# Attention with the values as TensorE weights: the transposed output, normalised and gated behind the product

## The chip, the cores and the metric

The kernel runs on one core of a Trainium2 chip. The metric is the device time of one execution in microseconds (us), lower is better. All data are float32 in HBM at the start and at the end. TensorE multiplies (a matmul is a load of its stationary operand, the weights, and the pass of the moving one), VectorE and ScalarE work elementwise and read PSUM, GpSimd gathers and scatters, SyncE issues most DMAs. Each engine takes its instructions in program order and meets the others at semaphores.

## What is computed

Three layers one after the other: chunked attention with memory, then two mixtures of experts. The part that the change touches is the attention and the first gate:

```python
B, H, S, D = 4, 8, 768, 64          # chunk 32, 16 keys to the left, 8 to the right, 8 memory keys
for c in range(S // 32):            # per chunk: 32 queries against its 56 keys and the 8 of memory
    scores = scale * np.matmul(q_c, k_full.transpose(0, 1, 3, 2))
    a = np.exp(scores - np.max(scores, axis=-1, keepdims=True))
    a = a / (np.sum(a, axis=-1, keepdims=True) + 1e-09)
    out[:, :, c_start:c_end] = np.matmul(a, v_full)
x = out.transpose(0, 2, 1, 3).reshape(3072, 512)
logits = x @ w_gate                 # 3072 x 8; tokens are then given to experts by sorted logits
```

The first mixture gives every expert 384 of the 3072 tokens in order of the logits; the second takes the best two experts of each token.

## The kernel before, in words

Attention goes in 32 blocks of 96 queries (8 for each of the 4 batch rows) against 128 keys: 120 of the context and 8 of memory, with a mask added by a matmul. `stages` runs `step(b, i, before, after)` for each block n = 8b + i; batch rows 0 and 3 are unrolled, rows 1 and 2 are a loop of 8 unrolled steps. The work is pipelined over blocks, in each engine by an order written out by hand:

- TensorE (lines 570 to 660), in the step of block n: `turn_probs(n)` for the two head parities (r = 0, 1), `scores(n+1)` (two mask matmuls at L594, then 16 matmuls at L600, two heads in different halves of the rows), `turn_x(n-1)` (4 transposes), `turn_qk(n+2)` (4 + 4 transposes), `sums(n)` (the value product: 16 matmuls at L612, the turned probabilities are the weights, 96 columns, and the values move, 64 columns; float32 takes two matmuls each), `gate(n-1)` (8 matmuls, the gate's 8 columns as weights, 96 columns moving).
- ScalarE (L1388 to L1426): `copy_logits(n-2)`, `copy_x(n-1)` out of PSUM, the 8 exponentials of block n+1 with their row sums, `copy_q(n+2)`.
- VectorE (L905 to L953): the two copies of the turned probabilities of n, the inverse of the row sums, the two maxima of n+1, `copy_k(n+2)`, `normalise(n)` of the sums of n into x.
- SyncE (L443 to L460): the load of block n+4, five DMAs, once the value product of n is done (a ring of 4 input buffers), then the store of x of block n to `x_dram`, once it is normalised. Before the loop it loads block 0, the two gates of the second mixture, the gate `gate_w`, and blocks 1 to 3.

Before its first scores TensorE waits for the masks and for the gate weights. After block 31 it turns the logits of all tokens, kept as 8 x 3072, in 24 transposes; VectorE copies them and the routing of the first mixture begins (L1092 and on). Ahead of its last `normalise` VectorE has a chain of constants for the routing (L982 to L997). The experts' weights, the routing and everything else come behind that and are not touched.

## Time and profile before

| | us |
|---|---|
| timed runs: median of 3 (lowest, highest) | 1430.89 (1430.78, 1433.11) |
| the profiled execution | 1426.65 |
| its span, first to last instruction | 1424.9 |
| granted TensorE clock, mean over the span | 0.94 |
| busy: TensorE matmul / weight load | 1268.4 / 1125.7 |
| busy: VectorE / ScalarE / GpSimd | 952.5 / 594.2 / 294.3 |

The busy time of a TensorE row is modelled at its end, since matmuls are pipelined; the distance between the starts of two groups is the better measure of what a group takes. The span has three stages: attention to about 193 us, the first mixture with its routing to about 700, the second to the end. The profile's clock is 1.00 where the granted clock is 2.4 GHz and 0.50 where it is 1.2 GHz.

### The profile page before, as it was taken

What the parts mean: (1) busy time and instruction counts of PE and PEld (TensorE: products, weight loads), DVE (VectorE), ACT (ScalarE), POOL (GpSimd) and SP (SyncE); (2) the same over time, 40 slices, a digit from 0 to 9 for tenths busy, and PEclk for the clock granted to TensorE, in tenths of its full rate; (3) what the DMA queues carried; (4) which work ended last, traced back from release to release, by engine and by line L of the source; (5) the groups of instructions that cost most, each with busy time, mean ns of one, the idle gap of its engine ahead of it and who ended that gap; (6) DMA issues with size and microseconds to landing.
All of it is one profiled execution on the core that took longest, in us unless ns stands there. A gap on an engine that the chain in (4) does not pass through costs nothing.

```text
span 1424.9 us, 28417 instructions
## 1 busy us (share of the span) xinstructions
PE 1268.4 (89%) x9825; PEld 1125.7 (79%) x9825; DVE 952.5 (67%) x1904; ACT 594.2 (42%) x1252; POOL 294.3 (21%) x345
## 2 busy tenths in 40 slices
PE   7999962599989999889249999999999999999997
PEld 6888851478778778768149999898989999999996
DVE  4777757788888787344666666666666666666662
ACT  4666621123323323333214545444445454444541
POOL 2000000210220210220122423332323333333322
PEclk9999975599999999899659999999999999999999
DMA  8888853133333233432013425124343324252110
GB/s 144 169 161 166 169 199 120 57 123 115 102 111 113 88 123 115 144 133 72 16 46 104 133 60 177 38 82 134 94 147 117 131 81 138 72 163 87 61 32 3
DMA packets 174760, 154.62 MB, mean 109 GB/s; under 512 B 105581, under 2 KB 138349, under 8 KB 174704
## 3 DMA queue, kind: packets, MB, share of 16 engines
q1 hardware_dynamic: 151552, 102.83, 26.2%
q0 software_dynamic: 16608, 44.56, 10.1%
q10 hardware_dynamic: 6544, 6.49, 1.3%
q8 instruction: 35, 0.57, 0.2%
q14 instruction: 21, 0.17, 0.0%
HBM read 215.58 MB, written 34.28 MB: 175 GB/s over the span
## 4 chain that ended last, share of the span: by engine, by line
issue 38%; PE 31%; DVE 12%; POOL 10%; DMA 6%; ACT 2%; POOLq 1%; DVEq 0%; SPq 0%; ACTq 0%
PE bank L730 6%; PE bank L750 5%; POOL partial L400 3%; DMA out<-result,token_now 3%; PE bank L612 3%; POOL out L404 3%; DMA xg<-x_dram,token_of 3%; PE bank L621 2%; PE bank L600 2%; POOL held L382 2%; PE bank L682 2%; POOL x L386 2%; PE bank L636 2%; PE bank L696 1%; PE bank L629 1%
## 5 line engine op out<-in xcount | busy, mean ns | idle before, releaser
L536 DVE TENSOR_TENSOR w_part<-w_sb,w_part 128x1024 fp32r<-128x1024 f32 x296 | 361.1, 1223 | 113.8 <-ACT w_part L530 105.4
L530 ACT CAST w_part<-w_sb 128x1024 fp32r<-128x1024 f32 x296 | 307.0, 1046 | 215.1 <-PE bank L890 169.7
L873 PEld LDWEIGHTS bank<-x2T,w_part 128*128 128x128 f32 x2784 | 339.2, 193 | 4.0 <-DVE x2T L1332 1.8
L873 PE MATMUL bank<-x2T,w_part 128*128 128x256 f32 x2784 | 340.1, 284 | 1.4 <-DVE x2T L1332 1.4
L890 PE MATMUL bank<-w_part,h2T 128*128 128x512 f32 x1392 | 323.2, 391 | 0.0
L890 PEld LDWEIGHTS bank<-w_part,h2T 128*128 128x128 f32 x1392 | 259.2, 188 | 52.6
L750 PE MATMUL bank<-w_part,hT 128*128 128x512 f32 x576 | 155.3, 409 | 8.2 <-DVE w_part L536 8.2
L730 PE MATMUL bank<-xgT,w_part 128*128 128x384 f32 x768 | 146.4, 345 | 2.6 <-DVE hT L1040 1.8
L356 POOL DMA_INDIRECT xg<-x_dram,token_of x24 | 32.6, 1358 | 554.9 <-DVE token_of L1071 302.5
L1544 ACT ACTIVATE h2T<-bank 128x512 fp32r<-128x512 f32 x116 | 69.3, 597 | 174.8 <-PE bank L873 174.8
L730 PEld LDWEIGHTS bank<-xgT,w_part 128*128 128x128 f32 x768 | 135.8, 192 | 5.0 <-DVE hT L1040 1.6
L1338 DVE SCALAR_TENSOR_TENSOR h2T<-bank,h2T 128x512 fp32r<-128x512 f32 x116 | 80.2, 692 | 86.0 <-ACT h2T L1544 86.0
L750 PEld LDWEIGHTS bank<-w_part,hT 128*128 128x128 f32 x576 | 103.4, 190 | 28.1 <-issue 9.7
L382 POOL TENSOR_TENSOR held<-iota_p 1x1 f32<-1x1 f32 x87 | 41.3, 475 | 406.7 <-DVE result L1357 388.3
L1392 ACT ACTIVATE probs<-bank,neg_max 96x128 f32<-96x128 f32 x256 | 89.3, 368 | 7.9 <-DVE neg_max L909 7.9
L1435 ACT ACTIVATE hT<-bank 128x384 fp32r<-128x384 f32 x64 | 31.5, 492 | 126.6 <-PE bank L730 126.6
L1357 DVE SCALAR_TENSOR_TENSOR result<-bank,w_now,partial 128x512 f32<-128x512 f32 x58 | 43.4, 748 | 44.8 <-PE bank L890 44.8
L386 POOL DMA_INDIRECT x<-y_dram,slot_now x58 | 60.9, 1050 | 56.0 <-DVE slot_now L1324 38.6
L682 PEld LDWEIGHTS bank<-above,proposal 128*8 128x8 bf16 x1176 | 31.8, 83 | 51.1 <-DVE above L1115 44.1
L682 PE MATMUL bank<-above,proposal 128*8 128x32 bf16 (+1 forms) x1176 | 37.5, 177 | 38.8 <-DVE above L1115 38.8
L400 POOL DMA_INDIRECT partial<-out,token_now x58 | 62.5, 1078 | 18.6 <-issue 16.2
L404 POOL DMA_INDIRECT out<-result,token_now x58 | 59.2, 1021 | 21.6 <-POOL held L382 16.0
(256 smaller groups left out, 1341.9 us busy)
## 6 DMA issues: line engine op xcount, KB each, us to landing
w_sb<-in_moe_w SPq DMA_DIRECT2D x296, 512.0 KB
k_in<-in_k SPq DMA_DIRECT2D x32, 240.0 KB
v_in<-in_v SPq DMA_DIRECT2D x32, 240.0 KB
q_in<-in_q SPq DMA_DIRECT2D x32, 192.0 KB
x_dram<-x_sb SPq DMA_DIRECT2D x32, 192.0 KB, 3.4
out<-zeros SPq DMA_DIRECT2D x1, 6144.0 KB, 19.7
y_dram<-y_sb ACTq DMA_DIRECT2D x24, 256.0 KB, 2.0
x<-y_dram,slot_now POOLq DMA_INDIRECT x58
```

The source lines that it names most:

```text
L386: pool.indirect_dma_start(out=x2[:, par, half, :], out_offset=None, in_=y_dram[:, :], in_offset=bass.IndirectOffsetOnAxis(ap=slot_now[:, p ...
L400: pool.indirect_dma_start(out=partial[:, par, half, :], out_offset=None, in_=out[:, :], in_offset=tokens[half], bounds_check=N - 1, oob_is ...
L404: pool.indirect_dma_start(out=out[:, :], out_offset=tokens[half], in_=result[:, par, half, :], in_offset=None, bounds_check=N - 1, oob_is_ ...
L530: scalar.copy(split_part(0, c), raw_part(c)).then_inc(hi_ready[c], 1)
L536: nc.vector.tensor_tensor(split_part(1, c), raw_part(c), split_part(0, c).bitcast(F32), ALU.subtract).then_inc(lo_ready[c], 1)
L682: last = nc.tensor.matmul(counts[:, 0:bins], proposal[:, c, :], above[:, c, 0:bins], start=(c == 0), stop=(c == COLS - 1))
L730: last = nc.tensor.matmul(bank[2 + f % 2][:, 0:CAP], w1_part[a][:, kt, f * P:(f + 1) * P], xgT[b][:, kt, :], start=(kt == 0 and n == 0), s ...
L750: last = nc.tensor.matmul(bank[4 + t % 2][:, :], hT[a_][:, f, t * P:(t + 1) * P], w2_part[b_][:, f, :], start=(f == 0 and n == 0), stop=(f ...
L873: last = nc.tensor.matmul(bank[2 + g % 2][:, at:at + TILE], w1_part[a][:, kt, f * P:(f + 1) * P], x2T[b][:, kt, :], start=(f % 2 == 0 and ...
L890: last = nc.tensor.matmul(bank[4 + half][:, :], h2T[a][:, f, half * P:(half + 1) * P], w2_part[b][:, f, :], start=(f == 0 and n == 0), sto ...
L1338: V.scalar_tensor_tensor(h2T[1][:, two_f, :].rearrange("p k s -> p (k s)"), bank[2 + g % 2][:], 0.0, h2T[0][:, two_f, :].bitcast(F32).rear ...
L1392: nc.scalar.activation(probs[:, r, j, :], ps_s[r][0:QB, j * P:(j + 1) * P], ACT.Exp, bias=neg_max[:, r, j:j + 1], accum_out=row_sum[:, i % ...
```

## The change

The value product swaps its operands. The values of one head are the weights (64 columns), the turned probabilities move (96 columns), and the two heads of a pair write PSUM partitions 0 to 63 and 64 to 127 by their tile position. The output of a block so comes out transposed, 128 features by 96 queries for each of 4 pairs, and not yet normalised. From there:

- ScalarE copies it to `xT` in the step of the block itself, last in its step. TensorE turns it back in the next step (4 transposes that move 128 columns), and VectorE normalises it out of that bank.
- The gate takes `xT` as weights (96 columns) and moves `gate_w`, now 16 columns a pair, each head's half of the rows beside zeros, and so gives the logits of each head apart: 96 x 8 x 8. VectorE multiplies them by the inverses and sums over heads (`gather_logits`). They share bank 0 with the turned q, so `gate(n-1)` waits for the copy of q of block n+2, and the turning of q for `gather_logits`.
- SyncE stores the logits of each block (96 x 8), to DRAM for batch rows 0 to 2 and into the routing's tile for the last, and reads the earlier ones back ahead of the last batch row. The 24 transposes and VectorE's copy of the logits go away.
- The copy of the turned k moves from VectorE to ScalarE, behind the exponentials; the copy of q moves ahead of them. On TensorE `turn_qk` comes ahead of `turn_x` and `gate`, and these ahead of `sums`.
- `gate_w` is cleared by GpSimd first, and loaded in two DMAs that stand behind the loads of blocks 1 to 3.
- The last `normalise` and `gather_logits` come ahead of VectorE's constants.

The diff, cut (semaphores, the memory layout's comments and a helper left out):

```diff
+        logits_dram = nc.dram_tensor("logits_dram", [N, E], F32)
...
+        ps_h = bank[0][:, 4 * QB:4 * QB + 8 * 8]
...
-        gate_w = asb("gate_w", [P, KT, E])
-        logitsT = asb("logitsT", [E, N])
+        gate_w = asb("gate_w", [P, KT, 2 * E])
+        head_logits = asb("head_logits", [QB, H, E])
+        block_logits = asb("block_logits", [QB, 2, E])
...
+            nc.gpsimd.memset(gate_w[:], 0.0).then_inc(gate_zeroed, 1)
...
-            sp.dma_start(gate_w[:], moe_w_gate.rearrange("(k p) e -> p k e", p=P)).then_inc(gate_loaded, 16)
             for i in range(1, RING):
                 load(0, i)
+            sp.wait_ge(gate_zeroed, 1)
+            for r in range(2):
+                rows = slice(64 * r, 64 * r + 64)
+                sp.dma_start(gate_w[rows, :, r * E:(r + 1) * E], moe_w_gate.rearrange("(k p) e -> p k e", p=P)[rows, :, :]).then_inc(gate_loaded, 16)
             def store_x(b, i):
                 sp.wait_ge(x_ready, b * BLOCKS + i + 1)
                 sp.dma_start(x_dram[bass.ds(b * S + i * QB, QB), :], x_sb[:, i % 2, :]).then_inc(x_stored[i % 2], 16)
+                sp.wait_ge(block_logits_ready, b * BLOCKS + i + 1)
+                if isinstance(b, int) and b == B - 1:
+                    place = logits[(b * BLOCKS + i) * QB // COLS:(b * BLOCKS + i + 1) * QB // COLS, :, :]
+                else:
+                    place = logits_dram[bass.ds(b * S + i * QB, QB), :]
+                sp.dma_start(place, block_logits[:, i % 2, :]).then_inc(logits_in[i % 2], 16)
...
+            for i in range(2):
+                sp.wait_ge(logits_in[i], 16 * (NT - BLOCKS) // 2)
+            done = (B - 1) * S
+            sp.dma_start(logits[0:done // COLS, :, :], logits_dram[0:done, :].rearrange("(p c) e -> p c e", c=COLS)).then_inc(old_logits_in, 16)
...
+                wait_pos(head_logits_up, n - 3)
...
             def sums(b, i):
                 n = b * BLOCKS + i
-                wait_pos(x_ready, n)
+                wait_pos(xT_copied, n)
                 for r in range(2):
                     pe.wait_ge(probs_copied[r], n + 1)
-                    for j in range(PAIRS):
+                for j in range(PAIRS):
+                    for r in range(2):
                         h = 2 * j + r
-                        last = nc.tensor.matmul(ps_o[0:QB, h * D:(h + 1) * D], probsT[:, r, j, :],
-                                                v_in[:, i % RING, h * D:(h + 1) * D], start=(h == 0), stop=(h == H - 1))
+                        rows = slice(64 * r, 64 * r + 64)
+                        last = nc.tensor.matmul(ps_o[rows, j * QB:(j + 1) * QB], v_in[:, i % RING, h * D:(h + 1) * D], probsT[:, r, j, :],
+                                                start=(j == 0), stop=(j == PAIRS - 1), tile_position=(0, 64 * r))
                 last.then_inc(pv_ready, 1)
             def turn_probs(b, i, r):
...
                     last = nc.tensor.transpose(ps_p[r][:, j * QB:(j + 1) * QB], probs[:, r, j, :], ident[0:QB, 0:QB])
                 last.then_inc(probs_turned[r], 1)
-            def turn_x(n, par):
-                pe.wait_ge(x_ready, n + 1)
-                wait_pos(xT_copied, n)
-                wait_pos(logits_copied, n)
+            def gate(n):
+                if isinstance(n, int) and n >= NT - 3:
+                    pe.wait_ge(q_copied, NT)
+                else:
+                    pe.wait_ge(q_copied, n + 4)
+                wait_pos(head_logits_up, n)
                 for j in range(KT):
-                    last = nc.tensor.transpose(ps_x[:, j * QB:(j + 1) * QB], x_sb[:, par, j * P:(j + 1) * P], ident[0:QB, 0:QB])
+                    last = nc.tensor.matmul(ps_h[0:QB, j * 2 * E:(j + 1) * 2 * E], xT[:, j, :], gate_w[:, j, :], start=(j == 0), stop=(j == KT - 1))
+                last.then_inc(head_logits_ready, 1)
+
+            def turn_x(n):
+                pe.wait_ge(xT_copied, n + 1)
+                wait_pos(x_ready, n)
+                for j in range(KT):
+                    last = nc.tensor.transpose(ps_x[0:QB, j * P:(j + 1) * P], xT[:, j, :], ident[:])
                 last.then_inc(x_turned, 1)
-
-            def gate(n):
-                pe.wait_ge(xT_copied, n + 1)
-                wait_pos(logits_copied, n)
-                for j in range(KT):
-                    last = nc.tensor.matmul(ps_x[0:E, KT * QB:(KT + 1) * QB], gate_w[:, j, :], xT[:, j, :], start=(j == 0), stop=(j == KT - 1))
-                last.then_inc(logits_ready, 1)
             def step(b, i, before, after):
                 n = b * BLOCKS + i
...
                     turn_probs(b, i, r)
                 if after >= 1:
                     scores(*later(b, i, 1))
-                if before >= 1:
-                    turn_x(n - 1, (i - 1) % 2)
                 if after >= 2:
                     turn_qk(*later(b, i, 2))
+                if before >= 1:
+                    turn_x(n - 1)
+                    gate(n - 1)
                 sums(b, i)
-                if before >= 1:
-                    gate(n - 1)
             pe.wait_ge(const_step, IDENT_OPS)
             turn_qk(0, 0)
             pe.wait_ge(const_step, CONST_OPS)
-            pe.wait_ge(gate_loaded, 16)
+            pe.wait_ge(gate_loaded, 16 * 2)
             scores(0, 0)
             turn_qk(0, 1)
             stages(pe, step)
-            turn_x(NT - 1, 1)
+            turn_x(NT - 1)
             gate(NT - 1)
-
-            pe.wait_ge(logits_copied, NT)
-            for c in range(COLS):
-                last = nc.tensor.transpose(bank[0][:, c * E:(c + 1) * E], logitsT[:, c:N:COLS], ident[0:E, 0:E])
-            last.then_inc(logits_turned, 1)
...
-            def copy_k(b, i):
-                dve.wait_ge(k_turned, b * BLOCKS + i + 1)
-                nc.vector.tensor_copy(kT[:, i % 2, :, :].rearrange("p j s -> p (j s)"), ps_k[:]).then_inc(k_copied, 1)
...
-            def normalise(b, i, n):
-
+            def normalise(b, i):
+
+                n = b * BLOCKS + i
                 dve.wait_ge(inv_step, 2 * n + 2)
                 if not (isinstance(n, int) and n < 2):
                     dve.wait_ge(x_stored[i % 2], 16 * (b * (BLOCKS // 2) + i // 2))
-                dve.wait_ge(pv_ready, n + 1)
+                dve.wait_ge(x_turned, n + 1)
                 nc.vector.tensor_tensor(x_sb[:, i % 2, :].rearrange("p (h d) -> p h d", h=H),
-                                        ps_o[0:QB, :].rearrange("p (h d) -> p h d", h=H),
+                                        ps_x[0:QB, :].rearrange("p (h d) -> p h d", h=H),
                                         row_inv[:, i % RING, :].unsqueeze(2).to_broadcast([QB, H, D]), ALU.mult).then_inc(x_ready, 1)
+            def gather_logits(b, i):
+
+                n = b * BLOCKS + i
+                if not (isinstance(n, int) and n == 0):
+                    dve.wait_ge(block_logits_ready, n)
+                dve.wait_ge(head_logits_ready, n + 1)
+                nc.vector.tensor_tensor(head_logits[:], ps_h[0:QB, :].rearrange("p (h e) -> p h e", h=H),
+                                        row_inv[:, i % RING, :].unsqueeze(2).to_broadcast([QB, H, E]), ALU.mult).then_inc(head_logits_up, 1)
+                if not (isinstance(n, int) and n < 2):
+                    dve.wait_ge(logits_in[i % 2], 16 * (b * (BLOCKS // 2) + i // 2))
+                dve.wait_ge(head_logits_up, n + 1)
+                nc.vector.tensor_reduce(block_logits[:, i % 2, :], head_logits[:].rearrange("p h e -> p e h"), AX.X, ALU.add).then_inc(block_logits_ready, 1)
+
             def step(b, i, before, after):
-                n = b * BLOCKS + i
                 for r in range(2):
                     copy_probs(b, i, r)
                 invert(b, i)
                 if after >= 1:
                     for r in range(2):
                         maxima(*later(b, i, 1), r)
-                if after >= 2:
-                    copy_k(*later(b, i, 2))
-                if not (isinstance(b, int) and b == B - 1 and i == BLOCKS - 1):
-                    normalise(b, i, n)
-
-            copy_k(0, 0)
+                if before >= 1:
+                    normalise(*last_block(b, i))
+                    gather_logits(*last_block(b, i))
+
             for r in range(2):
                 maxima(0, 0, r)
-            copy_k(0, 1)
             stages(dve, step)
-
+            normalise(B - 1, BLOCKS - 1)
+            gather_logits(B - 1, BLOCKS - 1)
...
-            normalise(B - 1, BLOCKS - 1, NT - 1)
             dve.wait_ge(route_consts, 1)
-            dve.wait_ge(logits_turned, 1)
-            link(V.tensor_copy(logits[:].rearrange("p c e -> p (c e)"), bank[0][:, 0:COLS * E]))
+            for i in range(2):
+                dve.wait_ge(logits_in[i], 16 * NT // 2)
+            dve.wait_ge(old_logits_in, 16)
...
+            def copy_k(b, i):
+                act.wait_ge(k_turned, b * BLOCKS + i + 1)
+                nc.scalar.copy(kT[:, i % 2, :, :].rearrange("p j s -> p (j s)"), ps_k[:]).then_inc(k_copied, 1)
+
             def copy_x(n):
-                act.wait_ge(x_turned, n + 1)
-                nc.scalar.copy(xT[:].rearrange("p j s -> p (j s)"), ps_x[:, 0:KT * QB]).then_inc(xT_copied, 1)
-
-            def copy_logits(n):
-                act.wait_ge(logits_ready, n + 1)
-                nc.scalar.copy(logitsT[:, bass.ds(n * QB, QB)], ps_x[0:E, KT * QB:(KT + 1) * QB]).then_inc(logits_copied, 1)
+                act.wait_ge(pv_ready, n + 1)
+                if not (isinstance(n, int) and n == 0):
+                    act.wait_ge(head_logits_ready, n)
+                nc.scalar.copy(xT[:].rearrange("p j s -> p (j s)"), ps_o[:, 0:KT * QB]).then_inc(xT_copied, 1)
             def step(b, i, before, after):
                 n = b * BLOCKS + i
-                if before >= 2:
-                    copy_logits(n - 2)
-                if before >= 1:
-                    copy_x(n - 1)
+                if after >= 2:
+                    copy_q(*later(b, i, 2))
                 if after >= 1:
                     for r in range(2):
                         exps(*later(b, i, 1), r)
                 if after >= 2:
-                    copy_q(*later(b, i, 2))
+                    copy_k(*later(b, i, 2))
+                copy_x(n)
             copy_q(0, 0)
+            copy_k(0, 0)
             for r in range(2):
                 exps(0, 0, r)
             copy_q(0, 1)
+            copy_k(0, 1)
             stages(act, step)
-            copy_logits(NT - 2)
-            copy_x(NT - 1)
-            copy_logits(NT - 1)
...
-            act.wait_ge(logits_turned, 1)
+            act.wait_ge(x_ready, NT)
+            act.wait_ge(block_logits_ready, NT)
+            for i in range(2):
+                act.wait_ge(logits_in[i], 16 * NT // 2)
...
```

## Rows read from the trace of the kernel before

**Rows 1.** Busy time by stretch: us, PE, PEld, DVE, ACT, POOL, clock, DMA, GB/s

```profile
30.00:60.00 30.00, 29.94 (x337) 26.15 (x334) 21.84 (x43) 19.82 (x101) 0.00 (x0) 1.00 0.85 171
...
300.00:330.00 30.00, 27.21 (x284) 21.12 (x283) 24.82 (x69) 11.67 (x19) 6.20 (x6) 1.00 0.27 85
```

**Rows 2.** Waits, 30 to 180 us: engine, line, releaser: total, times, longest

```profile
PEld bank L621 <- ACT probs L1392: 5.3, 27, 0.2
```

**Rows 3.** One block in order of time: start us, us, instruction, count, idle before

```profile
96.11 0.12 PEld L594 LDWEIGHTS bank<-window,chunk_of 64*96 64x96 bf16 x2
...
97.33 0.36 PEld L629 LDWEIGHTS bank<-ident,x_sb 96*128 96x128 f32 x4
...
97.44 1.28 DVE L909 TENSOR_REDUCE neg_max<-bank 96x4 f32<-96x512 f32 x2 [0.35 <-PE bank L600]
97.64 0.39 PEld L579 LDWEIGHTS bank<-ident,q_in 96*128 96x128 f32 x4
...
97.92 0.48 ACT L1401 COPY xT<-bank 128x384 f32<-128x384 f32 x1 [1.89 <-PE bank L629]
97.97 0.44 PEld L582 LDWEIGHTS bank<-ident,k_in 128*128 128x128 f32 x4
...
98.30 0.37 ACT L1392 ACTIVATE probs<-bank,neg_max 96x128 f32<-96x128 f32 x1
98.38 1.46 PEld L612 LDWEIGHTS bank<-v_in,probsT 128*96 128x96 f32 x16
...
99.91 0.59 PEld L636 LDWEIGHTS bank<-xT,gate_w 128*8 128x8 f32 x8
...
100.15 0.32 SPq L426 DMA_DIRECT2D q_in<-in_q  x1
...
100.67 0.36 PEld L621 LDWEIGHTS bank<-ident,probs 96*128 96x128 f32 x4 [0.17 <-issue]
...
100.96 0.22 ACT L1392 ACTIVATION_READ_ACCUMULATOR probs<-bank,neg_max 96x1 f32 x1
101.05 0.50 ACT L1397 ACTIVATE qT<-bank 128x384 f32<-128x384 f32 x1
101.23 0.36 PEld L621 LDWEIGHTS bank<-ident,probs 96*128 96x128 f32 x4 [0.20 <-ACT probs L1392]
...
101.71 0.42 PE L594 MATMUL bank<-window,chunk_of 64*96 64x512 bf16 x2
```

**Rows 4.** The first microseconds in order of time

```profile
9.12 0.69 DVE L905 COPY kT<-bank 128x512 f32<-128x512 f32 x1 [9.12 <-PE bank L582]
...
9.96 0.66 PE L594 MATMUL bank<-window,chunk_of 64*96 64x512 bf16 x2 [0.88 <-DVE kT L905]
...
15.30 1.13 SPq L430 DMA_DIRECT2D v_in<-in_mem_v  x1
```

**Rows 5.** Busy time by stretch of half a microsecond, same columns as rows 1

```profile
18.50:19.00 0.50, 0.50 (x8) 0.34 (x4) 0.00 (x0) 0.00 (x0) 0.00 (x0) 1.00 0.05 9
...
105.50:106.00 0.50, 0.50 (x7) 0.49 (x7) 0.28 (x1) 0.50 (x5) 0.00 (x0) 1.00 0.45 147
```

**Rows 6.** DMA issues: target, engine, count, KB each, median us to landing

```profile
y_dram<-y_sb ACTq DMA_DIRECT2D x24, 256.0 KB, 2.0
...
gate_w<-in_moe_w_gate SPq DMA_DIRECT2D x2, 16.0 KB, 3.6
```

**Rows 7.** Groups by line and form, 0 to 340 us: busy, mean ns, idle before

```profile
L1446 ACT COPY y_sb<-bank 128x512 f32<-128x512 f32 x3 | 1.8, 587 | 7.1 <-PE bank L750 7.1
```

**Rows 8.** The end of attention in order of time

```profile
191.49 1.50 PE L612 MATMUL bank<-v_in,probsT 128*96 128x64 f32 x16
...
192.15 0.12 DVE L984 COPY digit_bits<-digit_bits 128x32 uint32<-128x32 uint32 x1
...
195.08 0.69 DVE L931 TENSOR_TENSOR x_sb<-bank,row_inv 96x512 f32<-96x512 f32 x1
...
202.25 0.36 DVE L1092 TENSOR_TENSOR work<-logits,limit 128x192 f32<-128x192 f32 x1
```

More of the change, by code:

```diff
@@ L225, in build @@
         xT_copied = sem("xT_copied")
-        logits_ready = sem("logits_ready")
-        logits_copied = sem("logits_copied")
-        logits_turned = sem("logits_turned")
+        gate_zeroed = sem("gate_zeroed")
+        head_logits_ready = sem("head_logits_ready")
+        head_logits_up = sem("head_logits_up")
+        block_logits_ready = sem("block_logits_ready")
+        logits_in = [sem(f"logits_in{i}") for i in range(2)]
+        old_logits_in = sem("old_logits_in")
         zeros_up = sem("zeros_up")
@@ L563, in later, with last_block @@
             return b + (i + by) // BLOCKS, (i + by) % BLOCKS
+        def last_block(b, i):
+            return (b, i - 1) if i else (b - 1, BLOCKS - 1)
         @block.tensor
```

## The prediction

> **What bounds the kernel now.** I read first the table of busy time by stretches [rows 1]. In attention (the first 193 us) TensorE is busy 29.94 of 30 us at granted clock 1.00, the 2.4 GHz level; read alone, it says that every nanosecond taken off TensorE's list comes off the time. The view of waits says otherwise [rows 2]: in each of the 27 blocks of that stretch the weight loads of the probability transposes stood still until ScalarE's exponentials were ready, 5.3 us in all. So I went through one block in order of time [rows 3], counted from its mask matmul at 96.11; the next starts at 101.71, a period of 5.60 us. A ring of waits gives exactly that: scores take until the first maximum starts, +1.33; two maxima take 1.28, so the first is done near +1.97; ScalarE first copies the turned x (97.92, +1.81) and starts the exponentials behind it at 98.30 (+2.19); the last accumulator read ends at 101.18 (+5.07); the second group of probability transposes, which waited 0.20 for it, starts at 101.23 (+5.12); the next block's mask matmul follows at +5.60. The rest of TensorE's work lies beside the exponentials: turning x 0.31, q 0.33, k 0.41, value sums 1.53, gate sums 0.76 (differences of the starts in rows 3), then the first four probability transposes, 0.36. It is done 0.20 us before it is needed. TensorE looks full because its ends are modelled and its gaps are short; the ring TensorE, VectorE, ScalarE, TensorE sets the pace.
>
> **The change part by part.** Times are against the profiled execution, 1426.65 us (span 1424.9); the median of the timed runs is 1430.89, so my differences go onto that at the end.
>
> *Value sums, x and gate on TensorE.* The 16 matmuls of the value sums took 1.53. With 64 weight columns and 96 moving ones they cost between 0.76, if the two heads of a pair run side by side, and 1.53, if they do not and nothing is gained. Turning x now moves 128 columns, as turning k does: 0.41 for 0.31, +0.10. The gate loads 96 weight columns and moves 16: eight at the price of the value sums' pace (1.53 / 16) are 0.77, for 0.76. In the new order TensorE reaches the first probability transposes at 1.22 + 0.31 (q) + 0.41 (k) + 0.41 (x) + 0.77 (gate) + 0.76 to 1.53 = 3.88 to 4.65 and is through with four of them at 4.24 to 5.01, still ahead of +5.12. The effect is **zero at either end**: what the value sums save is idle time. The gate now waits for the copy of q out of the bank that they share: it is called for at +2.35 and the copy, started like today's copy of x at +1.81 and 0.50 long [rows 3], ends at +2.31. That fits.
>
> A rule of the Trainium skill speaks against the change here: "TensorEngine Tiling (Array Packing)", Key Properties, says that a change of tiling mode, not of tile alone, drains the array. The change adds two such switches a block. If each took the 0.17 us that stands idle ahead of the transposes at 100.67 [rows 3], the upper end would come to 5.35 and pass +5.12 by 0.23: 28 x 0.23 = 6.4 us more than my sum; at the lower end, 4.58, it stays hidden. No row shows a column-tiled matmul.
>
> *ScalarE.* The copy of q takes the place of the copy of x ahead of the exponentials. Both follow four transposes of 96 columns begun at +1.22, and the copy of x lets the next instruction start after 0.38: the exponentials start at +2.19 as before. **Zero.** But the copy of k moves from VectorE to the place behind the exponentials, and the next scores wait for it. It can start at 101.05 (+4.94), where the copy of q starts now; a 128x512 copy on ScalarE is 0.587 [rows 7]; it ends at +5.53. What follows such a copy is shown once: the copy of k of the first block ended at 9.81 and the mask matmul started at 9.96, 0.15 later [rows 4]. So scores start at +5.68 and not +5.60: 0.08 a block, bounds 0 (the copy does end before +5.60) and 0.20 (the length of the one such stall in rows 3, should the sequencer have to work through the waits behind it). 28 steady blocks: **+2.2 us** (0 to 5.6). Below zero is not possible here, since nothing in the ring gets shorter. The copy of x then ends near +6.0, and ScalarE is wanted at +7.4.
>
> *VectorE.* It loses the 0.69 of k and gains two small operations on 96x64; normalising comes a block later. It is free from +2.6 (maxima) to +4.3 at the earliest (first probability copy); 0.69 plus two of at most 0.3 each fit. Zero. If that cover is gone it delays the probability copies, which have over 2 us before the value sums.
>
> *The start.* This is the largest term. TensorE waits for the gate weights ahead of its first scores. Their DMA was the third issue after the first block's load; now two DMAs stand behind the loads of blocks 1 to 3 on SyncE. The last of those issues starts at 15.30 and takes 1.13, to 16.43 [rows 4]. The second gate DMA so goes out near 16.9, and gate weights landed 3.6 us after their issue [rows 6]: 20.5. The data of the loads ahead have drained by 18.5 to 19 [rows 5], so it is not under 19.2. I take 20.3. The first mask matmul started at 9.96 [rows 4], so attention starts **10.3 us later** (9.2 to 11). Nothing hides it: TensorE has only the first q and k turned and nothing else that goes ahead of that wait. The clearing of the gate tile on GpSimd, ahead of the other constants, is covered by the same wait.
>
> At the start TensorE is slow (the mask pair took 0.66, and 0.42 at 101.71). There the q transposes and their copy ahead of the exponentials are longer than the maxima: 0.5 us a block for the two blocks before it is at pace: **+1.0** (0 to 2).
>
> *SyncE.* Stores and logits of block n wait for work of block n+1; a pass through the list has seven DMAs where it had six, of 0.32 to 1.13 us each [rows 3, 4], some 4.3 us at their middle, my estimate, in 5.6: it fits. At the turn to the last batch SyncE waits for the landing of logits of block 23, behind which the load of block 28 is queued, and TensorE waits for that load. Loads go out at +4.04 (100.15, rows 3) and their data end near 105.9 [rows 5], +9.8, wanted at 12.4: 2.6 us of room. The logits go out near +9.5 of block 23, land 2.0 to 3.6 later [rows 6], the load then starts at 12 to 13.5 in place of 9.6: 2.4 to 3.9 late against 2.6 of room. **+1.0** (0 to 2).
>
> *The end.* Today the last value sums start at 191.49; VectorE goes through constants from 192.15 and normalises the last block only at 195.08; then turning, copying, gate, 24 transposes of logits, their copy; routing starts at 202.25 [rows 8]. After the change the sums end near 193.5, copy of x 0.6, turning 0.65, normalising 0.69, the two logit operations 0.5: 195.9. The constants (2.93 us, 192.15 to 195.08) come behind, to 198.9; beside them the last logits go out and land 2.0 to 3.6 us later, with the issue some 198.5 to 200. Routing starts near 199.3: **-3.0** (-1.5 to -4).
>
> Sum: 10.3 + 1.0 + 2.2 + 1.0 - 3.0 = **+11.5 us**. 1438.2 for the profiled execution; on the median 1430.9 + 11.5 = 1442.4, given as 1442. Adding the low ends gives +5.2 and the high ends +19.1, that is 1436 to 1450. All that follows attention runs on the router's chain and is only shifted.
>
> **The rivals.**
> *TensorE is the bound after all (faster).* For it: 29.94 of 30 us busy [rows 1]. Against: the 0.20 us of waiting in every block [rows 2]. If it holds, side-by-side heads save 0.77 - 0.11 = 0.66 a block, times 28 = -18.5, with +10.3 + 1.0 (SyncE) - 3.0 of the rest: -10.2, 1421. It decides where TensorE reaches the second group of probability transposes later than the exponentials do, +5.12. The same page of the skill, Overview, gives up to twice the speed for such pairs; the score pairs here, in different halves of the rows, do something like it: the mask pair and 16 matmuls of 128 columns take 1.22 [rows 3], where four transposes of 128 columns alone take 0.41.
> *The late gate weights cost nothing*, because the scores do not in fact stand behind them or the start-up is made good later: the sum without 10.3 and the 1.0 is +0.2, 1431. Against: the wait stands ahead of the first scores in program order, and the ring has no reserve to make good.
> *The clock falls.* With shorter value sums TensorE idles up to 0.9 us in each block. If it drops to the 1.2 GHz level, some 5 us of work take 9 to 10, about +4 a block until it recovers; three such blocks give +12, 1454. Against: at 27.21 busy of 30 the granted clock was 1.00 [rows 1].
>
> **How the numbers follow.** Forecast 0.73; TensorE-bound 0.09; start hidden 0.07; clock 0.11. A measurement here can tell about 0.2%, 3 us, from no change. Faster 0.09, same 0.07, slower 0.84. The range is the forecast's own, widened by 1 below and 3 above towards the clock case: 1435 to 1453; outside it lie the two cases below (0.16) and little above.
>
> **What would show it.** First scores near 20 us and a TensorE wait on a DMA or an issue gap of some 10 us ahead of them; a period of 5.6 to 5.8 with value sums of 0.8 to 1.5 us and a longer wait than 0.20 for the exponentials; the mask matmul about 0.15 behind the copy of k; one stall near block 26; routing 3 us closer to the last value sums. A period below 5.5 would refute the ring, first scores before 15 us the largest term.

## The result, and the profile after

The changed kernel took 1442.9 us (median of 5 timed runs, 1441.11 to 1443.87), the kernel before 1433.11 (5 runs on the same chip, 1430.78 to 1435.6): a ratio of 1.007, 95% interval 1.0054 to 1.0087. It is slower by 9.8 us. The forecast was 11.5 us slower and 1442. The profiled execution has a span of 1439.2 us for 1424.9, 14.3 more; why this is more than the timed difference is a finding of its own, below.

The change took work off TensorE. Busy time by stretch in attention, columns as in rows 1, kernel after:

```profile
100.00:130.00 30.00, 27.08 (x334) 23.59 (x333) 19.95 (x49) 20.97 (x97) 0.00 (x0) 1.00 0.86 164
```

TensorE is busy 27.08 of 30 us, where it was 29.94 [rows 1], at the same granted clock of 1.00; and no block is shorter for it. One block of the changed kernel in order of time, the counterpart of rows 3 (start us, us, instruction, count, idle before):

```profile
122.83 0.15 PEld L617 LDWEIGHTS bank<-window,chunk_of 64*96 64x96 bf16 x2
...
124.08 0.36 PEld L602 LDWEIGHTS bank<-ident,q_in 96*128 96x128 f32 x4
124.16 1.28 DVE L926 TENSOR_REDUCE neg_max<-bank 96x4 f32<-96x512 f32 x2 [0.36 <-PE bank L623]
124.39 0.45 PEld L605 LDWEIGHTS bank<-ident,k_in 128*128 128x128 f32 x4
...
124.67 0.49 ACT L1425 ACTIVATE qT<-bank 128x384 f32<-128x384 f32 x1 [1.53 <-PE bank L602]
124.80 0.46 PEld L663 LDWEIGHTS bank<-ident,xT 128*96 128x96 f32 x4
...
125.05 0.35 ACT L1420 ACTIVATE probs<-bank,neg_max 96x128 f32<-96x128 f32 x1
125.23 0.78 PEld L656 LDWEIGHTS bank<-gate_w,xT 128*96 128x96 f32 x8
...
126.04 0.69 PEld L637 LDWEIGHTS bank<-probsT,v_in 128*64 128x64 f32 x16
...
126.86 0.36 PEld L646 LDWEIGHTS bank<-ident,probs 96*128 96x128 f32 x4
...
127.69 0.22 ACT L1420 ACTIVATION_READ_ACCUMULATOR probs<-bank,neg_max 96x1 f32 x1
127.79 0.60 ACT L1429 COPY kT<-bank 128x512 f32<-128x512 f32 x1
127.96 0.37 PEld L646 LDWEIGHTS bank<-ident,probs 96*128 96x128 f32 x4 [0.74 <-ACT probs L1420]
...
128.46 0.15 PEld L617 LDWEIGHTS bank<-window,chunk_of 64*96 64x96 bf16 x2
```

The value sums take 0.82 (126.04 to 126.86) for 1.53 in rows 3: two heads do run side by side. The first probability transposes are reached at +4.03 (126.86 - 122.83) in place of +4.56. But the exponentials start at +2.22, as before at +2.19, and the wait for them ahead of the second transposes has grown from 0.20 to 0.74 us. The period is 5.63 us for 5.60. The view of waits adds them up, 37 to 175 us, the counterpart of rows 2:

```profile
PEld bank L646 <- ACT probs L1420: 18.7, 25, 0.8
```

What the value product saved stands there as idle time. The chain of what ended last tells the same, and shows a trap. In a stretch of 30 us of the kernel before, and then of the kernel after, it gives (shares by line):

```profile
by line: PE bank L612 22.2%; PE bank L621 20.6%; PE bank L636 15.1%; PE bank L600 14.6%; PE bank L629 8.0%; PE bank L582 7.3%; PE bank L594 6.9%; PE bank L579 5.5%; issue 0.2%
```

```profile
by line: ACT probs L1420 49.0%; PE bank L623 14.6%; PE bank L646 10.2%; PE bank L602 8.2%; ACT qT L1425 6.7%; PE bank L617 6.4%; issue 5.6%; ACTq L1434 0.1%
```

Before, nearly all of it was TensorE, and the value sums led with 22%; the likely reason, not shown by a run, is that the modelled end of one row covered the short gap ahead of the next. Nearly half the value sums' time was then taken away, and the exponentials, which had been part of the pacing work all along, came into view.

The start, counterpart of rows 4, in order of time, and the landing of the gate weights, counterpart of rows 6:

```profile
16.08 1.40 SPq L448 DMA_DIRECT2D gate_w<-in_moe_w_gate  x2
```

```profile
19.35 0.66 PE L617 MATMUL bank<-window,chunk_of 64*96 64x512 bf16 x2 [10.29 <-DMA gate_w<-in_moe_w_gate]
```

```profile
gate_w<-in_moe_w_gate SPq DMA_DIRECT2D x2, 8.0 KB, 2.6
```

TensorE stood 10.29 us for the gate weights, which nothing needs before the second step, and started its first scores at 19.35 and not at 9.96. The second of the two DMAs went out at 16.89 and landed 2.4 us later, near 19.3. The turn to the last batch, in order of time:

```profile
166.58 0.36 SPq L458 DMA_DIRECT2D logits_dram<-block_logits  x1
170.15 0.34 SPq L470 DMA_DIRECT2D logits<-logits_dram  x1
170.54 0.42 SPq L432 DMA_DIRECT2D q_in<-in_q  x1
```

```profile
176.63 0.37 PEld L602 LDWEIGHTS bank<-ident,q_in 96*128 96x128 f32 x4 [1.91 <-DMA v_in<-in_mem_v]
```

SyncE waited 3.0 us (its own view of waits) for 3 KB of logits to land, with the load of block 28 behind it, and TensorE then 1.91 us for that load. The end of attention, counterpart of rows 8:

```profile
204.41 1.51 PE L637 MATMUL bank<-probsT,v_in 128*64 128x96 f32 x16
...
206.50 1.09 PE L663 MATMUL bank<-ident,xT 128*96 128x128 f32 x4 [0.57 <-ACT xT L1435]
...
209.16 0.26 DVE L964 TENSOR_REDUCE block_logits<-head_logits 96x8 f32<-96x64 f32 x1
209.35 0.17 DVE L1012 COPY digit_bits<-digit_bits 128x32 uint32<-128x32 uint32 x1
...
212.41 0.36 DVE L1120 TENSOR_TENSOR work<-logits,limit 128x192 f32<-128x192 f32 x1
```

Routing starts at 212.41, 10.16 us later than before. The constants of 209.35 to 212.4 and not the DMA of the last logits end last here.

The granted clock had fallen while the last value sums ran: it was 1.00 in 202 to 204 us, 0.62 in 204 to 206, and then the lower of its two levels, 1.2 GHz. The last transposes and the last gate ran at that level:

```profile
206.00:208.00 2.00, 1.50 (x9) 1.48 (x9) 0.28 (x1) 0.44 (x1) 0.00 (x0) 0.50 0.25 68
```

### The profile page after: what moved, and what is told of

Same layout as the page of the kernel before. It is cut to its first block, busy times and chain, and to the rows that moved or that the text cites. A ratio compares the mean times of both kernels' runs of the same rounds, so it can differ in the third digit from the quotient of the medians.

```text
span 1439.2 us, 28595 instructions
## 1 busy us (share of the span) xinstructions
PE 1252.0 (87%) x9801; PEld 1112.7 (77%) x9801; DVE 946.8 (66%) x1935; ACT 605.8 (42%) x1252; POOL 295.7 (21%) x346
## 4 chain that ended last, share of the span: by engine, by line
issue 38%; PE 23%; DVE 12%; POOL 9%; ACT 8%; DMA 7%; SPq 1%; POOLq 1%; DVEq 0%; ACTq 0%
PE bank L751 6%; ACT probs L1420 5%; PE bank L771 5%; DMA out<-result,token_now 3%; POOL partial L406 3%; POOL out L410 3%; DMA xg<-x_dram,token_of 3%; PE bank L623 2%; POOL held L388 2%; PE bank L703 2%; POOL x L392 2%; PE bank L717 1%; PE bank L646 1%; DVE above L1143 1%; PE bank L602 1%
```

## The experiments

Theory: a ring through the exponentials paces the blocks, so TensorE's gain is worth nothing, and the loss comes from the gate weights at the start. Rivals: TensorE is the bound; the start is made good later or has another cause. All marks below are read in the traces, one execution each: start of the first mask weight load, median distance between two blocks' mask loads, the longest block behind the first two, start of the last block's scores and of routing, and the length of the first mixture from its first routing step to the first weight load of the second (the second's routing, from about 700 us on, is in it). The ratio compares the timed runs with those of the kernel before that were made beside them (their median was 1432.8 to 1436.0 us).

| run | first scores | period | longest | last scores | routing | mixture 1 | timed ratio to before (95%) |
|---|---|---|---|---|---|---|---|
| before | 9.93 | 5.60 | 5.60 | 185.66 | 202.25 | 536.60 | 1 |
| after | 19.32 | 5.63 | 7.39 | 197.90 | 212.41 | 539.93 | 1.007 (1.0054 to 1.0087) |
| e1_gate_early | 9.65 | 5.63 | 7.14 | 187.90 | 200.83 | 545.16 | 0.9994 (0.9975 to 1.0012) |
| e2_late_read | 20.40 | 5.63 | 5.80 | 198.09 | 212.76 | 540.47 | 1.0067 (1.0047 to 1.0087) |
| e3_both | 9.71 | 5.63 | 5.80 | 187.28 | 200.23 | 541.14 | 0.997 (0.9951 to 0.9988) |
| e7_short_ring | 9.64 | 5.46 | 5.54 | 181.56 | 197.29 | 544.22 | 0.9947 (0.9926 to 0.9967) |
| b1_gate_late | 19.98 | 5.59 | 5.60 | 195.48 | 211.93 | 548.47 | 1.0091 (1.0067 to 1.0116) |
| e4_sums_twice | 19.98 | 5.64 | 10.79 | 202.84 | 216.45 | 540.77 | 1.009 (1.0063 to 1.0116) |
| e5_heads_apart | 20.37 | 5.63 | 7.62 | 199.98 | 213.29 | 543.14 | 1.008 (1.0055 to 1.0104) |
| e6_k_vector | 20.05 | 5.60 | 6.40 | 195.28 | 209.78 | 546.62 | 1.0078 (1.0059 to 1.0097) |
| before_again | 10.01 | 5.60 | 5.60 | 184.32 | 200.67 | 548.99 | 0.9989 (0.9963 to 1.0015) |
| after_again | 19.97 | 5.63 | 9.68 | 201.64 | 214.57 | 555.62 | 1.0074 (1.0051 to 1.0098) |

**e1_gate_early.** The two DMAs of the gate weights go ahead of the loads of blocks 1 to 3.

```diff
+            sp.wait_ge(gate_zeroed, 1)
+            for r in range(2):
+                rows = slice(64 * r, 64 * r + 64)
+                sp.dma_start(gate_w[rows, :, r * E:(r + 1) * E], ...).then_inc(gate_loaded, 16)
             for i in range(1, RING):
                 load(0, i)
-            sp.wait_ge(gate_zeroed, 1)
-            for r in range(2):
...
```

> The changed kernel with the two DMAs of the gate weights issued ahead of the loads of blocks 1 to 3. My theory (the late gate weights hold the first scores): first mask matmul near 10 us in place of 19.35, everything behind it earlier by 9.4, so 1442.9 - 9.4 = 1433.5 us. The rival (the gate weights are not what holds it, the loads or the masks are, or attention makes the delay good elsewhere): first scores move, but the end of attention by under 3 us, 1440 to 1443.

The first scores moved to 9.65, the last to 187.90, 10.0 earlier, and the time to 1432.9 (median), no longer to be told from the kernel before. The start is the whole measurable loss.

```profile
9.68 0.66 PE L617 MATMUL bank<-window,chunk_of 64*96 64x512 bf16 x2 [0.77 <-ACT kT L1429]
```

In place of the 10.29 us for the gate weights this matmul waits 0.77 for the copy of k.

**b1_gate_late.** The converse, one part of the change alone in the kernel before: its gate DMA behind the loads.

```diff
-            sp.dma_start(gate_w[:], ...).then_inc(gate_loaded, 16)
             for i in range(1, RING):
                 load(0, i)
+            sp.dma_start(gate_w[:], ...).then_inc(gate_loaded, 16)
```

> The kernel before, with one part of the change alone: its one DMA of the gate weights stands behind the loads of blocks 1 to 3. My theory (TensorE's wait for the gate weights is the start-up term, and nothing later makes it good): first mask matmul at about 19 us in place of 9.96, the rest shifted by as much, slower by 9 us, ratio 1.0063. The rival (the delay comes from other parts of the new start): same as before within 0.2%.

```profile
20.01 0.66 PE L594 MATMUL bank<-window,chunk_of 64*96 64x512 bf16 x2 [10.67 <-DMA gate_w<-in_moe_w_gate]
```

The same wait, 10.67 us, in a kernel with nothing else of the change. The first scores come 10.05 later than before and routing 9.68 later, so attention makes almost none of it good. The timed ratio, 1.0091 (9.6 to 16.7 us), lies above the 9 us forecast, and has the 9.68 of the trace at its low end.

**e2_late_read.** SyncE's wait for the earlier logits, and their reading back, stand behind the last load.

```diff
-            for i in range(2):
-                sp.wait_ge(logits_in[i], 16 * (NT - BLOCKS) // 2)
-            done = (B - 1) * S
-            sp.dma_start(logits[0:done // COLS, :, :], ...).then_inc(old_logits_in, 16)
             for i in range(BLOCKS):
                 if i < BLOCKS - RING:
                     sp.wait_ge(pv_ready, (B - 1) * BLOCKS + i + 1)
                     load(B - 1, i + RING)
+                if i == BLOCKS - RING:
+                    for side in range(2):
+                        sp.wait_ge(logits_in[side], 16 * (NT - BLOCKS) // 2)
...
```

> The changed kernel with the reading back of the earlier logits, and SyncE's wait for them, four blocks later, behind the load of block 31. My theory (the load of block 28 stands behind that wait): the one block of 7.35 us in the trace becomes 5.63, 1442.9 - 1.7 = 1441.2 us. The rival (the DMA engines are full there and the load comes late by itself): the long block stays, 1442.9.

The long block is gone (longest 5.80). The transposes of block 28's q wait for nothing:

```profile
176.80 0.37 PEld L603 LDWEIGHTS bank<-ident,q_in 96*128 96x128 f32 x4
```

In the time it does not show: 1443.8 beside 1434.7 of before, a ratio of 1.0067 for 1.007. This execution's first scores came at 20.40, 1.1 later than in the trace of after: SyncE issued the gate DMAs 0.67 later (16.75) and the second landed 2.8 us after its issue for 2.4. The trace settles the cause, the timing cannot.

**e3_both.** Both edits. 

> The changed kernel with both edits: gate weights early and the reading back late. If the terms add as my sum has them: 1442.9 - 9.4 - 1.7 = 1431.8 us; that is 0.999 of the kernel before. What is left of the change is then +0.9 of a longer period, +0.3 of the loop ends and -2.1 at the end of attention. If the terms overlap (one stall hides the other): 1433.5 or more.

1431.6 us, as forecast (1431.8); the ratio is 0.997 where 0.999 was forecast. What then remains of the change is a small gain. In the trace routing starts 2.0 us earlier than before, 0.4 earlier than in before_again; by the marks the gain stems from the end of attention (12.94 us from the last scores to routing, for 16.59).

**e4_sums_twice.** The value product of every block is made twice; nothing is left out.

```diff
+                for again in range(2):
-                for j in range(PAIRS):
-                    for r in range(2):
+                    for j in range(PAIRS):
+                        for r in range(2):
...
```

> The changed kernel with the value product of each block made twice (the second pass begins its sums anew, so the result is the same): 0.81 us more of TensorE's work in each of 32 blocks. My theory (the ring paces; the weight loads of the second probability transposes now wait 0.75 for the exponentials): about 0.75 of the 0.81 disappears in that wait, the period grows by 0.06 to 0.15, +2 to +5 us, 1445 to 1448. The rival (TensorE is the bound): +0.81 x 31 = +25 us, 1468.

```profile
104.84 1.54 PE L638 MATMUL bank<-probsT,v_in 128*64 128x96 f32 x32
...
106.31 0.82 PEld L647 LDWEIGHTS bank<-ident,probs 96*128 96x128 f32 x8
```

The value sums take 1.48 (104.83 to 106.31), the wait ahead of the second transposes is used up (eight transposes in one row), and the period is 5.636 for 5.627, no more than the 5.635 of e2 and e3, where the sums are made once. Some 0.66 us of TensorE work more in each block costs at most 0.009 us: TensorE is not the bound. The timed median, 1447.1, is 11.2 us over that of the kernel before beside it; for the change it was 9.8, and 12.6 in after_again. So the second product costs nothing that the timing can tell, and not the 25 us that the rival wanted.

The one long block, 10.79 for 7.39, is another matter, and mostly not of the load. From its mask loads to its q transposes, which stand behind the load, it took 3.4 us, where after took 3.0. Behind that stall the granted clock stood at 0.50 until 185.5, and the double value sums took 2.76 us (182.27 to 185.03) for 1.48:

```profile
182.00:184.00 2.00, 2.00 (x25) 1.96 (x26) 0.51 (x3) 1.26 (x7) 0.00 (x0) 0.50 0.34 98
```

The same happened in after_again, the change itself (9.68, clock 0.50 from 178 to 185), where that first stretch took 3.1 us; in after, with 3.0, the clock stayed at 1.00. So this part came with and without the second product, and it is the prediction's third rival in small.

**e5_heads_apart.** The loops over pairs and halves exchanged, so that all matmuls of one half come first.

```diff
-                for j in range(PAIRS):
-                    for r in range(2):
+                for r in range(2):
+                    for j in range(PAIRS):
```

> The changed kernel with the value product's two loops exchanged: all matmuls of one half of the output's partitions, then all of the other, so that heads of a pair no longer stand side by side. If the array works on two column tiles at once only when they alternate, the value product goes from 0.81 us to about 1.3 (16 x 0.082). By the ring the time stays at 1442.9 all the same (0.75 of room); if TensorE is the bound it grows by 0.5 x 31 = 15 us. If the value product stays at 0.81 the gain does not come from alternating.

```profile
105.13 1.07 PEld L637 LDWEIGHTS bank<-probsT,v_in 128*64 128x64 f32 x16
...
106.32 0.36 PEld L646 LDWEIGHTS bank<-ident,probs 96*128 96x128 f32 x4
```

1.19 us for 0.82: the gain comes from two column tiles in turn. The period stays (5.635) and the time too (ratio 1.008), so neither the good nor the bad order of the value product is worth anything here.

**e6_k_vector.** The copy of k back on VectorE, ahead of `normalise`.

```diff
 (scalar)
-                if after >= 2:
-                    copy_k(*later(b, i, 2))
                 copy_x(n)
 (vector)
                         maxima(*later(b, i, 1), r)
+                if after >= 2:
+                    copy_k(*later(b, i, 2))
```

> The changed kernel with the copy of the turned k back on VectorE, behind the maxima; everything else as in the change. My theory (the copy of k on ScalarE is what holds the scores by 0.03 a block and by some 0.15 at the two loop ends): the period goes from 5.63 back to 5.59 or 5.60, about -1.2 us in all, 1441.7, which the profile can show and the timing hardly. The rival (the 0.03 comes from elsewhere, such as switches of TensorE's tiling mode): period 5.63 as before.

The period is back at 5.596 and the two blocks of 5.79 at the ends of the loop are gone: both came from the scores' wait for ScalarE. The 1.2 us are inside the timing's noise: the median was 1446.7, beside a kernel before of 1436.0. One of its blocks, whose exponentials start at +2.19:

```profile
99.34 0.42 PE L617 MATMUL bank<-window,chunk_of 64*96 64x512 bf16 x2
...
101.53 0.35 ACT L1428 ACTIVATE probs<-bank,neg_max 96x128 f32<-96x128 f32 x1
...
104.94 0.42 PE L617 MATMUL bank<-window,chunk_of 64*96 64x512 bf16 x2
```

**e7_short_ring.** e3 and e6, and the ring cut: the copy of q behind the exponentials, the gate's sums in bank 6.

```diff
-        ps_h = bank[0][:, 4 * QB:4 * QB + 8 * 8]
+        ps_h = bank[6][:, 4 * QB:4 * QB + 8 * 8]
...
 (gate)
-                    pe.wait_ge(q_copied, n + 4)
+                    pe.wait_ge(probs_copied[1], n + 2)
...
 (turn_probs)
+                if r == 1:
+                    wait_pos(head_logits_up, n - 1)
...
 (scalar)
-                if after >= 2:
-                    copy_q(*later(b, i, 2))
                 if after >= 1:
                     for r in range(2):
                         exps(*later(b, i, 1), r)
+                if after >= 2:
+                    copy_q(*later(b, i, 2))
```

> Both edits of the run before, and a shorter ring: the copy of k back on VectorE, the copy of q behind the exponentials, the gate's sums in another bank (beside the second group of turned probabilities) so that they need not wait for the copy of q. Nothing on TensorE gets shorter. My theory (the ring scores, first maximum, exponentials, probability transposes paces the blocks): the exponentials start right behind the first maximum, 0.12 to 0.16 earlier, the period falls from 5.63 to about 5.45, times 28 is 5.0: 1431.8 - 5.0 = 1426.8 us. The rival (TensorE's work paces the blocks): the period stays near 5.6, 1431 to 1432.

```profile
110.58 0.42 PE L617 MATMUL bank<-window,chunk_of 64*96 64x512 bf16 x2
...
111.91 1.28 DVE L932 TENSOR_REDUCE neg_max<-bank 96x4 f32<-96x512 f32 x2 [0.35 <-PE bank L623]
...
112.63 0.36 ACT L1430 ACTIVATE probs<-bank,neg_max 96x128 f32<-96x128 f32 x1 [1.84 <-DVE neg_max L932]
...
116.05 0.42 PE L617 MATMUL bank<-window,chunk_of 64*96 64x512 bf16 x2
```

The exponentials start at +2.05, behind the first maximum and no copy, and the period is 5.46. Beside e6 (+2.19 and 5.60), which already has the copy of k on VectorE, 0.14 off the start of the exponentials gave 0.14 off the period, with TensorE's work as it was: this shows the ring directly. The last scores start 5.7 us earlier than in e3, 5.0 of it by the period.

Routing starts only 2.9 earlier: from the last scores to routing it took 15.73 us for 12.94 in e3, and the granted clock was at 0.50 from about 187 on, ahead of the last value sums:

```profile
188.00:190.00 2.00, 2.00 (x19) 1.96 (x20) 1.26 (x4) 0.00 (x0) 0.00 (x0) 0.50 0.15 38
```

1428.9 us, ratio 0.9947 (0.9926 to 0.9967), where 1426.8 was forecast. It is the lowest median of all kernels here and beats both kernels of this document. That it is faster than e3 in time is not shown, since the two intervals overlap.

**before_again and after_again.** Both kernels unchanged. 

> The kernel before, unchanged, once more, for its trace. The profiles so far say that attention ends where the terms put it, but that the first mixture, whose instructions no run changes, takes from 536.6 us (before) to 548.5 us from its first routing step to the first weight load of the second mixture. If that length is drawn anew in each execution, this trace shows another length than 536.6, by some us, at the same start of routing, 202.3. If it is fixed by the kernel's own timing, it is 536.6 within 0.5.

 

> The changed kernel, unchanged, once more, for its trace. As for the run before: a first mixture other than 539.9 us by over 1 us says that its length is drawn anew in each execution, and that the 14.3 us between the two profiled spans are 10.2 of the change and the rest of chance; the same 539.9 says that it follows from the kernel. Attention's marks stay: first scores 19.3 to 20.4, period 5.63, routing starts near 212.5.

Not all marks of attention stayed. Routing started at 200.67 and not at 202.3 in before_again, since its first two blocks took 12.0 us for 13.4, and at 214.57 and not near 212.5 in after_again, because of the long block of 9.68. Attention itself is thus drawn anew by 1.6 to 2.2 us.

The first mixture's instructions are the same in all runs, and its length was 536.60 and 548.99 us in two executions of the kernel before, 539.93 and 555.62 in two of the kernel after. Its whole stretch in the four (us, PE, PEld, DVE, ACT, POOL, clock, DMA share, GB/s), before, before_again, after, after_again:

```profile
202.25:738.85 536.60, 403.77 (x3418) 341.46 (x3418) 384.73 (x1065) 151.17 (x247) 70.12 (x57) 0.86 0.32 106
```

```profile
200.67:749.66 548.99, 414.58 (x3417) 350.99 (x3418) 387.72 (x1065) 151.24 (x247) 70.65 (x57) 0.83 0.32 103
```

```profile
212.41:752.34 539.93, 406.28 (x3418) 344.04 (x3418) 387.31 (x1065) 151.02 (x247) 70.21 (x57) 0.85 0.33 107
```

```profile
214.57:770.19 555.62, 421.66 (x3417) 357.52 (x3417) 388.48 (x1065) 151.20 (x247) 70.80 (x57) 0.82 0.32 104
```

The longer it is, the lower its mean granted clock, 0.86, 0.85, 0.83, 0.82, and the longer the same TensorE instructions took. The clock falls between its two levels in this stage at places that differ from one execution to the next (in 350 to 400 us it was 1.00 in before and 0.83 in before_again). What decides where is open. So of the 14.3 us between the first two profiled spans, 10.2 belong to attention, 3.3 to the first mixture, well within its draw, and 0.9 to the second.

## Why the prediction was right, step by step

Direction, size and range held, and the reason for the forecast held too: the largest term is the start, and the ring hides what TensorE saves. That the sum came so close is in part luck. Three terms (start, first blocks, steady blocks) came out about 1 us lower each, two (SyncE's wait, the end) nearly 1 us higher each, and these errors cancel but for 1.3. The terms, in the two traces that the prediction and the result rest on:

| term | predicted | measured |
|---|---|---|
| first scores | +10.3 (9.2 to 11) | +9.39 (9.93 to 19.32); 10.0 to 10.5 in the five other changed runs with the late gate weights |
| two blocks below pace | +1.0 (0 to 2) | -0.1 (13.43 to 13.31, first scores to the third); +2.0 between the two repeats (12.00 to 13.97) |
| 28 steady blocks | +2.2 (0 to 5.6) | +0.9, and +0.3 at the two loop turns |
| SyncE's wait | +1.0 (0 to 2) | +1.8; 0.8 to 2.0 in e6, e1 and e5; 4.1 and 5.2 in after_again and e4, with the clock at 0.50 behind the stall |
| end of attention | -3.0 (-1.5 to -4) | -2.1 (16.59 to 14.51); -3.7 in e1, e3 and after_again |
| to the start of routing | +11.5 | +10.16 |

- **The bound.** Right: TensorE's 29.94 of 30 us was no bound. e4, e5 and e7 show it from three sides.
- **Value sums, x and gate.** The value sums came out at 0.82, close to the lower end of 0.76 to 1.53; TensorE reached the transposes at +4.03 for 3.88 to 4.65. All parts together overran the lower end by 0.15 (the value sums by 0.06, the gate by 0.04, the scores by 0.03, turning x by 0.02), and the wait ahead of the transposes, 0.74, hides it. By that, the Trainium skill's rule on mode switches ("TensorEngine Tiling (Array Packing)", Key Properties), weighed in the prediction at 0.17 a switch, finds no room for two such switches; the rule itself was not measured alone.
- **ScalarE.** The copy of q took the place of the copy of x to within 0.03. The copy of k ended at 128.39, 0.03 later in the block than forecast, and the mask matmul started at 128.49: 0.10 behind it, where the prediction took 0.15 from the one row at the start, when TensorE was slow. The term was mis-sized by that, not its mechanism; e6 removed it.
- **The start.** Right in mechanism, 0.9 too large: the second gate DMA went out at 16.89, as forecast (16.9), but landed 2.4 us later and not in the 3.6 of rows 6. The two carry half the bytes each.
- **The slow first blocks.** Not borne out between the two traces, and open beyond them. Between these two traces the term is -0.1, between the two repeats +2.0. What the rows show is when TensorE was fast. In after four probability transposes took 0.55 us at 23.99, the full pace, but then the granted clock fell to 0.50 from 27.0 to about 30.5, and four q transposes took 0.90 at 27.90:

```profile
27.00:29.00 2.00, 2.00 (x17) 1.72 (x14) 1.06 (x2) 0.16 (x1) 0.00 (x0) 0.50 0.00 0
```

  In before it was slow from the start (four q transposes 0.90 at 19.11, although the view gives a clock of 1.00 there), in before_again fast from 14.69 on. A fall of the clock shows there in e1, e2 and e5 too, and in no trace with the copy of k on VectorE (before, before_again, b1, e6, e7). Those five took 12.0 to 13.4 us for the two blocks, the seven others 13.2 to 14.0. Whether the changed start brings the clock down is not shown.
- **SyncE's wait.** The place and the mechanism held to the block. The load went out 3.4 us late (170.54 for 167.15 by the pace), within the 2.4 to 3.9 forecast, but the room was 1.6 us and not 2.6. The bound of 2 did not hold where the clock fell behind the stall (after_again, e4); the stall itself was there longer by 0.1 and 0.4 us only.
- **The end.** The logits did land beside the constants. But the gain was 2.1 where 3.0 was forecast, for two reasons. Turning x and the gate now stand ahead of the last value sums, so these start 6.5 us behind the last scores for 5.8, which the sum left out. And the clock had fallen: the four transposes took 1.09 us. In e1 and e3, where the same four took 0.64 and the clock fell only behind them, the gain was 3.7; in e2 and e6, where it fell as early as in after, 1.9 and 2.1.
- **The clock rival.** It held for no steady block: at 27.08 busy of 30 us the clock was 1.00. But it fell at three places of attention where TensorE had stood still or half idle: in the second block, behind the load of block 28, and at the end. Behind the load it cost after_again 2.2 us beside after, at the end it cost after 1.6 us beside e1.
- **What the sum did not hold**: the first mixture as "only shifted". It is shifted, and drawn anew by up to 12 to 16 us. The timed medians come from several executions each, and agree with the sum where the two profiled spans do not.

## What to carry to other kernels

An engine that is busy for 99.8% of a stage need not bound it: look for the wait that is left in each period, however short, follow the ring that it belongs to, and ask whether the edit shortens that ring. A saving off the ring turns into idle time, whereas a DMA reordered past others on its queue, or a wait put ahead of a load on an in-order queue, is paid as far as nothing behind it has slack: 10 us of the gate weights in full, 1.8 of the 3.4 us by which the one load was late. And compare stage by stage, with the granted clock of the stretch beside each difference: two profiled spans of this kernel differ by more from chance in one untouched stage than the change is worth.

## What was not expected of the hardware

- Column-tiled matmuls with 64 weight columns and 96 moving ones go at 0.051 us each when the two tiles alternate (0.82 / 16), and at 0.074 when they come one tile after the other (1.19 / 16).
- A 3 KB store held the engine that waited for its landing 3.0 us, in the range of 192 KB stores (median landing 3.4 in the profile before, 2.4 in this one).
- The same code of the first mixture took 536.6 to 555.6 us in four executions of two kernels, with a mean granted clock of 0.86 to 0.82.
- Behind one wait for a load the granted clock fell to 0.50 for some 6 us in two executions (after_again, e4) and stayed at 1.00 in a third (after); TensorE's wait was 2.00, 2.31 and 1.91 us, the block 9.68, 10.79 and 7.39 us.
